# Transposes two tiles behind the scores, products with V in the last two slots of the next head

## What is computed

```python
# q, k, v: (4, 8, 576, 64); U (576, 32), V (32, 576), w_ch1 (512, 2048), w_ch2 (2048, 512)
q_rot, k_rot = rotate(q), rotate(k)                       # rotary embedding
scores = 1/sqrt(64) * q_rot @ k_rot.transpose(0, 1, 3, 2)
scores = scores - max(scores)                             # over keys
attn = exp(scores);  attn = attn / (sum(attn) + 1e-9)
x = (attn @ v).transpose(0, 2, 1, 3).reshape(4, 576, 512)
u = x + ((x.transpose(0, 2, 1) @ U) @ V).transpose(0, 2, 1)
out = u + relu(u @ w_ch1) @ w_ch2
```

## Time and profile before

| | us |
|---|---|
| median of 3 runs (lowest, highest) | 828.53 (827.82, 830.4) |
| span of the profiled execution, first to last instruction | 826.5 |
| TensorE busy in the span | 747.6, 90% |
| VectorE, ScalarE, GpSimd busy | 379.0, 377.8, 259.9 |
| mean granted TensorE clock | 0.986 of full speed |

### The profile page before, as it was taken

How to read it: one execution, slowest core, us unless ns; L and a number is a source line. 1 busy time by engine, 2 the same in 40 slices (tenths; PEclk the granted TensorE clock), 3 DMA queues, 4 the chain that set the end, 5 groups by cost and what they waited for, 6 DMA issues and landing times.

```text
span 826.5 us, 12614 instructions
## 1 busy us (share of the span) xinstructions
PE 747.6 (90%) x4816; PEld 664.3 (80%) x4816; DVE 379.0 (46%) x645; ACT 377.8 (46%) x831; POOL 259.9 (31%) x182
## 2 busy tenths in 40 slices
PE   0799989899898989883999999999999999999998
PEld 0688979788777988762988888888878888888886
DVE  2689887879877877775111123111141111321112
ACT  1699988889878987754222311111111112111110
POOL 6677768655865676002433310000000000000000
PEclk9999999999999999997899999999999999999999
DMA  7856655576468743445522103100013000030001
GB/s 238 236 159 184 205 159 159 153 216 196 111 171 228 190 123 84 121 140 167 201 92 77 52 1 104 69 1 1 1 55 118 1 1 1 0 115 1 1 1 58
DMA packets 43419, 86.55 MB, mean 105 GB/s; under 512 B 7584, under 2 KB 16992, under 8 KB 40800
## 3 DMA queue, kind: packets, MB, share of 16 engines
q1 hardware_dynamic: 42928, 84.50, 34.9%
q10 hardware_dynamic: 432, 1.25, 0.4%
HBM read 43.25 MB, written 14.16 MB: 69 GB/s over the span
## 4 chain that ended last, share of the span: by engine, by line
PE 51%; DVE 1%; ACT 0%; issue 0%; DVEq 0%
PE ps L867 26%; PE ps L852 25%; DVE utl L806 1%; DVE res L813 1%; ACT hth L797 0%; ACT wh L776 0%; DVE wl L817 0%; DVE htl L825 0%; DVEq L812 0%
## 5 line engine op out<-in xcount | busy, mean ns | idle before, releaser
L825 DVE SCALAR_TENSOR_TENSOR htl<-ps,hth 128x288 fp32r<-128x288 f32 x128 | 58.5, 458 | 349.0 <-ACT hth L797 349.0
L797 ACT ACTIVATE hth<-ps 128x288 fp32r<-128x288 f32 x128 | 52.6, 412 | 347.7 <-PE ps L852 347.7
L852 PE MATMUL ps<-uth,wh 128*128 128x288 f32 x512 | 152.5, 298 | 11.5 <-DVE utl L806 11.5
L852 PE MATMUL ps<-uth,wl 128*128 128x288 f32 x512 | 152.5, 298 | 0.0
L852 PE MATMUL ps<-utl,wh 128*128 128x288 f32 x512 | 152.3, 297 | 0.0
L614 PE MATMUL ps<-stack 128*128 128x288 f32 (+1 forms) x640 | 124.5, 317 | 22.3 <-DMA stack<-raw 22.3
L508 DVE TENSOR_REDUCE negmax<-ps 128x1 f32<-128x576 f32 (+1 forms) x160 | 120.3, 752 | 52.6 <-PE ps L614 51.3
L424 ACT ACTIVATE prob<-ps,negmax 128x576 f32<-128x576 f32 (+1 forms) x160 | 118.4, 740 | 40.6 <-DVE negmax L508 40.0
L867 PE MATMUL ps<-wh,hth 128*128 128x512 f32 (+1 forms) x320 | 125.2, 391 | 5.0 <-DVE res L813 5.0
L867 PE MATMUL ps<-wh,htl 128*128 128x512 f32 (+1 forms) x320 | 125.2, 391 | 0.0
L867 PE MATMUL ps<-wl,hth 128*128 128x512 f32 (+1 forms) x320 | 125.1, 391 | 0.0
(11 more groups left out here) (63 smaller groups left out, 888.0 us busy)
## 6 DMA issues: line engine op xcount, KB each, us to landing
stack<-raw SPq DMA_DIRECT2D x192, 144.0 KB, 2.6
raw<-in_qk SPq DMA_DIRECT2D x16, 1152.0 KB, 5.5
tables<-in_w SPq DMA_DIRECT2D x16, 512.0 KB, 3.6
raw<-scratch_ut SPq DMA_DIRECT2D x4, 1152.0 KB, 7.6
vraw<-in_v SPq DMA_DIRECT2D x16, 256.0 KB, 5.4
scratch_u<-xn SPq DMA_DIRECT2D x16, 256.0 KB, 3.3
scratch_ut<-uts SPq DMA_DIRECT2D x16, 256.0 KB, 3.4
res<-scratch_u SPq DMA_DIRECT2D x16, 256.0 KB, 3.8
```

Of the source, the lines that this page charges most:

```text
L797: nc.scalar.activation(hth[:, i % 2, CH * c:CH * c + CH], ps[:, up_bank(j):up_bank(j) + CH], ACT.Relu).then_inc(relu_hi, 1)
L825: nc.vector.scalar_tensor_tensor(htl[:, i % 2, CH * c:CH * c + CH], ps[:, up_bank(j):up_bank(j) + CH], 0.0, hth[:, i % 2, CH * c:CH * c + CH],
L852: mm = nc.tensor.matmul(ps[:, up_bank(j):up_bank(j) + CH], l[:, f, 0, P * d:P * d + P], r[:, CH * c:CH * c + CH], start=(d == 0 and q == 0 ...
```

## The change

`LAG` goes from 1 to 2, so the transposes of tile n are made in slot n + 2; ScalarE's rounded copy and VectorE's subtraction move with them, and so does the order in which the ring's banks are taken. Half 0 of the product with V goes from slot t2 of the next head to t3; half 1 stays in t4. The number of `prob` buffers (`NP = NT + 1 = 6`), of ring banks (4) and of score buffers (2), and the slots of the mixing steps stay. The blank lines at the head of the file are dropped too.

```diff
-LAG = 1
+LAG = 2
...
-PV_START = {2: 0, 4: 1}
-PV_END = {2: 0, 4: 1}
+PV_START = {3: 0, 4: 1}
+PV_END = {3: 0, 4: 1}
```

## The result

The changed kernel takes 833.79 us in the median of 4 runs (833.22 to 834.98), against 829.46 (827.82 to 831.37) for the kernel before, in 4 runs beside them: a ratio of 1.0056, with a 95% interval of 1.0037 to 1.0075. It is slower by 4.3 us, where 9.1 were to be won, and 0.8 us above the forecast range. Lines of the changed file are 17 lower than before: scores L597, product L580, transposes L615 and L610, exponential L407, copy L416, lower half L423, maximum L491, subtraction L497, addition L505.

The account below looks back on a forecast made before the run. Attention alone could move, bound mostly by ScalarE in the first batch and by TensorE in slots 21 to 40. Terms summed to -10.6 us, with near ties -9.1, so 819.4 us, range 813 to 825 (chance 0.56).

Parts of the forecast that it names:

- near ties: In t4 slots transposes meet the bank of the preceding slot's product within 0.05 us; eight a batch at 0.06 each, +1.5 us.
- The product moved from t2 to t3: Two heavy TensorE slots in a row, 4.6 us, make exponential t1 to next t0 7.2 us: 0.3 a pair of new wait.
- Transposes one slot later: Scores no longer wait for the exponential, freeing the 5.29 us path t0 to t3; t1's maximum waits 0.32 to 0.44 a head.
- Start: In the cold first slots the scores of tile 2 start 0.8 us sooner and what is won lasts: -1.0 us.
- Where TensorE is the bound: Slots 21 to 40 of a batch with mixing: 7.0 of 46.4 us are waits; -2.5 a batch, -7.5 us in all.
- The low-rank wait: TensorE's 0.88 us wait for the low-rank result shrinks to 0.15, covered by scores, product and transposes of slots 22 and 23.
- two new waits of the list: New TensorE waits in mixed slots: about 1.0 us at slot 27, for tile t4's subtraction, and 0.6 at slot 31.
- The stall of slot 11: ScalarE's rope wait stays; TensorE's idle time shrinks from 2.39 to about 1.6 us, half clock vanishes: -2.1 us.
- Start and end: Besides the gain in the first slots, one more subtraction after tile 159 precedes the last head's product: +0.6 us.
- Six buffers, GpSimd, SP: Exponential t1 waiting for transposes, and the later roped K copy: both priced at nothing, at most 6 and 8 us.
- Ring, slower: Rival: t4 transposes wait for the bank of the product at t3, costing 16 us: 834 us; chance 0.18.
- No change: Rival: scores of t3 start 0.55 us after exponential t1, making the way to next t0 7.6 us: 829.0 us; chance 0.15.

Follow-up runs that it names:

- wait_late: Changed kernel with the product's wait for the last tile's subtraction moved three matmuls later, to the first matmul that needs it: 828.66 us, ratio 0.9991.
- product_only: Kernel before with only half 0 of the product moved from t2 to t3, transposes still one slot behind: 832.42 us, ratio 1.0038.
- const_15: Changed kernel with VectorE's three one-time subtractions on mixing constants moved from slot 6 to slot 15: 833.04 us, ratio 1.0058.
- mixes_light: wait_late with the residual and transposed mixing steps moved into slots without a product: 836.95 us, ratio 1.0106.
- natural_early: wait_late with mixing step `natural` 1, which feeds the chain to GpSimd's rope, moved from slot 8 to slot 7: 821.99 us, ratio 0.992.
- const_late: Changed kernel with VectorE's three one-time subtractions on mixing constants moved from slot 6 to slot 8, beside GpSimd's work: 834.6 us, ratio 1.0064.
- natural_spread: natural_early with VectorE's three one-time constant subtractions put one each into slots 16, 26 and 36 instead of slot 6: 823.07 us, ratio 0.9932.

## Why the prediction was wrong, by its own steps

Between forecast and result lie 13.4 us. The wait inside the product is the part that an experiment shows: wait_late takes 5.1 us of it back and makes "slower" into "no change". It doesn't make the change a gain; the largest miss in size is another, the slots where TensorE is the bound, where 6.0 us were forecast (7.5 less 1.5 for near ties) and 1.6 came.

**"The product moved from t2 to t3": the wait inside it was left out, 0.36 us in every slot t3, and it decides the sign.** The way from exponential t1 to t0 was put at 0.88 + 4.6 + 0.1 + 1.6 = 7.2 us. The 0.88 and the 1.6 are right to 0.02, and nothing delays the scores of t3. But I had taken a heavy slot as one block of 2.30 us. It has a wait in its middle, that of the second five matmuls for the lower parts of the whole head. With the product in t2 and a lag of one these parts were ready: the earlier trace rows show the slot at 2.41 with 0.11 of wait in all. With a lag of two they hang on the exponential t1 by way of two copies and two subtractions and end 2.37 us after its start, while the matmul could start after 2.17. The question to ask of each wait of the moved instruction was which exponential it now goes back to. The term was +0.1 a pair, measured were +0.75; wait_late takes it to +0.05 and so shows the cause. The pair, exponential by exponential (from the timelines, slots 20 to 30; the two values are for its two heads):

| | t0 to t1 | t1 to the next t0 | pair |
|---|---|---|---|
| before | 1.55, 1.56 | 7.38, 7.14 | 17.63 |
| wait_late | 1.62, 1.53 | 7.44, 7.10 | 17.69 |
| changed | 1.62, 1.87 | 7.45, 7.45 | 18.39 |
| product_only | 1.62, 1.87 | 7.49, 7.49 | 18.47 |

In the first head ScalarE's own work (7.4 us) hides the wait; there it shows only in the late t1 behind it, 1.87. In the second it lengthens the path itself, from 7.10 to 7.45.

**"Transposes one slot later": right where alone.** In wait_late the path is 7.10 and the pair 17.69, 0.06 above before, with 0.1 forecast. The order maximum, subtraction, maximum that I priced as a new wait of t1 was no new one: t1 came 1.56 us after t0 before and comes 1.62 after in one head, 1.87 in the other, where the late scores of t0 put VectorE's maximum, addition, subtraction and maximum in a row. In product_only it is the same, so this is not the later copy.

**"Start": right to slot 5, then wrong.** Beside exponential 0, exponential 5 comes 0.8 us sooner, as computed. The rest of the step, "what is won lasts", wasn't looked at: I moved the subtraction from slot 6 to 7 in the steady order and never listed what VectorE does once only. The constants stand between. That cost 2.7 us up to slot 10, a wait of 2.15 and a clock at half among them. const_15 shows that without them there, and with the clock at full, the start alone gives 2 us; but they cost as much elsewhere.

**"Where TensorE is the bound": right in direction, far off in size.** Forecast were -2.5 us a batch, with bounds 0 and -4.2. Measured are -0.5 (exponentials 60 to 80: 45.90 instead of 46.43 us; -0.5 in each of the others too). The step that failed first is the sum of TensorE's work, 39.4 us, with "7.0 us are waits". The trace of before has 4.5 us of waits in those slots (138.53 to 184.94; TensorE's waits of that window added up), so what stands between the waits is 41.9 us: 2.5 of the 7.0 were never there to win. In the changed kernel the same slots hold 3.2 us of waits and 42.7 us between them. The low-rank wait did what was said. TensorE's waits for that result from 22 to 390 us, all batches:

```profile
PE ps L646 <- DVE hs L542: 1.5, 1, 1.5
```

That is down from 4.1 us in four waits; the one left is at 378.41 in the rest of the last batch, as long as it was. In 140 to 185 us the wait is gone (0.88 before). The two new waits of the list came near their price: 0.33 + 0.40 at slot 27 (1.0 forecast) and 0.54 at slot 31 (0.6). With them, the waits for `ptl` in the twenty slots are 0.2 to 0.5 us each and 2.4 us in all, and each has a tail that I hadn't priced. TensorE in slot 23 of the batch:

```profile
149.99 0.40 PE L580 MATMUL ps<-pth,v 128*128 128x288 f32 x1 [0.28 <-DVE ptl L497]
150.23 0.30 PE L580 MATMUL ps<-ptl,v 128*128 128x288 f32 x1
150.36 0.29 PE L580 MATMUL ps<-pth,v 128*128 128x288 f32 x1
```

The matmul after the waiting one starts 0.24 us behind it instead of 0.13. The eight near ties that had been priced at 0.06 us each, transposes of t4 slots against the bank of the product, were the wrong ones: of them one wait of 0.09 us a batch shows (slot 34). What waits are products, mixes and other transposes, for banks or parts that a subtraction frees late. This much is a reading of the trace, not an experiment: mixes_light shows only that emptying the heavy slots doesn't help. Why 0.8 us more stand between the waits than before, and why ScalarE's forecast of 43.9 us wasn't reached, stays open.

**"The stall of slot 11": half right.** The rope is still waited for 2.4 us, as said. TensorE's idle time for the same exponential, now ahead of the scores of slot 14, shrinks to 1.24 us with 0.47 behind it, and the clock of the changed kernel is 1.00 from 124 to 128 us, as forecast. From exponential 50 to 60 this wins 0.96 us. But the slots 40 to 50 lose 0.85. Of that 0.36 are the wait inside the product, which wait_late takes back; 0.49 stay in wait_late and are open (TensorE's `natural` step in slot 6 of the batch waits 0.44 us there for a subtraction; no run moves that alone). So slots 0 to 20 of the three later batches come to -0.1, +0.5 and -0.2, where -3.0 had been forecast for all three. (+0.5 is the batch in which the kernel before kept its full clock.) natural_early shows what the stall itself was worth, 1.7 us a batch against wait_late, and it was open to the old order too.

**"Start and end", the end:** +0.6 forecast. From exponential 159 to the first product of the feed-forward part it is 32.13 us instead of 31.56, +0.6; another 0.3 lies in the feed-forward part, which the change leaves alone. **Six buffers, GpSimd, SP:** priced at nothing, and little found: from 22 to 390 us ScalarE's exponentials wait 2.1 us in all for transposes, 0.5 at most, and wait_late, with the same waits, is level with before in the first batch.

**The rivals.** "Ring, slower" came nearest in its time (834) and was not the cause: no transposes of the changed kernel wait more than 0.5 us for a bank. "No change" named the right place, the way from t1 to t0, and the right size, 7.6 against 7.45 measured, with another wait than the one that came. product_only is that rival to the letter. That its 834 was nearly the measured time is luck. The sign came from two waits on the same semaphore, in slot t3 and at the start, that none of my cases held; the large terms for TensorE's slots and for the stall stayed within their bounds, at the end of least gain.

## What to carry to other kernels

When a step is moved against the one that feeds it, list every wait inside it, at the instruction where it stands, and follow each back to the event that sets the pace: a slot is not a block. In an engine that works in order, a wait belongs ahead of the first instruction that needs it and not ahead of the group; three matmuls of 0.13 us were worth 5 us here. Before reckoning a gain as "length less work", add up the waits that the trace shows: a new order can win little more than these. And go through the one-time work in each queue a moved step crosses, since it stands in no steady-state row.

## What the runs showed of the hardware

- A subtraction with both operands in SBUF takes VectorE more than twice as long while GpSimd works on SBUF: 1.87 us instead of 0.81 for 128x640, and 1.86 instead of 0.77 each for the two of 32x576, with GpSimd's own instructions at 1.8 to 2.0 us instead of 1.41 (const_late against const_15). The subtractions of `ptl`, with one operand in PSUM, keep their 0.67 us beside it. The ends read like turns taken: GpSimd 40.83, VectorE 41.51, GpSimd 42.78, and in the end GpSimd 44.65, VectorE 45.26; each VectorE instruction ends 0.6 to 0.7 us after GpSimd's, about its length alone. The Trainium skill ("SBUF — State Buffer", section "Who interferes with whom") says that a VectorE instruction with two SBUF inputs contends with a GpSimd instruction that reads SBUF; the trace agrees.
- After a semaphore wait in the middle of a stream of matmuls of 288 columns the first is recorded with 0.40 us instead of 0.29, and the next starts after 0.24 instead of 0.13 (0.23 to 0.24 at 79.04, 149.99 and, in wait_late, 39.42). So a wait of 0.28 us costs 0.39.
- The length of one idle time doesn't tell alone whether the clock falls. It fell to 0.50 of full speed, within 2 us, after 1.93 us (natural_spread, slot 8), 2.15 (changed kernel, slot 8), and 2.39 and 2.41 (kernel before, slot 13 of the second and fourth batch). It stayed at 1.00 after 1.76 (wait_late, slot 8), 2.06 (kernel before, slot 8) and 2.42 (kernel before, slot 13 of the third batch), and after 1.24 with 0.47 behind it.
